# Top-32 attention and two feed-forward layers on one core: rows folded to pairs for the selection, a ScalarE mask, a transposed first layer, and unrolled loops

## The reference

```
scores = scale * np.matmul(q, k.transpose(0, 1, 3, 2))
kth    = np.partition(scores, -32, axis=-1)[..., -32:-31]
scores = np.where(scores >= kth, scores, -1e9)
attn   = np.exp(scores - max); attn = attn / (sum(attn) + 1e-09)
x      = (attn @ v), heads side by side: 2304 x 512
h      = x @ w_in;   y   = (h - tanh(h)) @ w_out            # first layer
h      = y @ w_in2;  out = where(h > 0, h, exp(min(h,0))-1) @ w_out2   # second layer
```

## Time and profile before

| | |
|---|---|
| median of 3 runs | 1284.04 us |
| profiled execution, first to last instruction | 1281.9 us (2.1 us under the median) |
| PE / PEld busy | 94% / 81% |
| DVE / ACT / POOL busy | 70% / 55% / 62% |
| second layer alone, from | 872 us |
| granted TensorE clock, mean | 0.98 |

### The profile page before, as it was taken

One profiled execution on the slowest core, in us unless ns is written; L12 is line 12 of the kernel. 1 busy time (PEld: TensorE's weight loads), 2 busy tenths in 40 slices (PEclk: granted clock), 3 DMA queues, 4 the chain that ended last, 5 costly groups with the idle time before them and its releaser, 6 DMA issues.

```text
span 1281.9 us, 23141 instructions
## 1 busy us (share of the span) xinstructions
PE 1203.8 (94%) x6784; PEld 1039.2 (81%) x6784; DVE 896.5 (70%) x1870; ACT 702.2 (55%) x1534; POOL 790.3 (62%) x579
## 2 busy tenths in 40 slices
PE   3678999999998999999999999999999999999997
PEld 2667887888887888888888888788888888888887
DVE  7999999999999999999999995015532222222221
ACT  5667777766776766777766765345432222222221
POOL 4898888888987888988888986332222222222221
PEclk9679999999999999999999999999999999999999
DMA  6410022000022100022000000504001001010000
GB/s 201 168 56 13 20 62 75 30 21 22 23 68 64 32 21 21 25 66 68 28 26 13 21 11 12 188 12 170 1 1 66 1 1 65 0 50 1 1 33 17
DMA packets 46420, 56.81 MB, mean 44 GB/s; under 512 B 13296, under 2 KB 28656, under 8 KB 45808
## 3 DMA queue, kind: packets, MB, share of 16 engines
q1 hardware_dynamic: 46320, 55.59, 13.7%
HBM read 45.61 MB, written 9.96 MB: 43 GB/s over the span
## 4 chain that ended last, share of the span: by engine, by line
PE 71%; issue 12%; DVE 6%; ACT 5%; POOL 4%; DVEq 0%; DMA 0%; ACTq 0%; POOLq 0%; SPq 0%
PE ps L683 15%; PE ps L728 15%; PE ps L611 11%; PE ps L626 10%; PE ps L598 9%; PE ps L579 4%; PE ps L563 2%; PE ps L564 2%; PE ps L653 2%; DVE best L973 1%; POOL keep L1104 1%; DVE work L1005 1%; DVE best L964 1%; PE ps L580 1%; ACT kT_hi_over_lo L755 1%
## 5 line engine op out<-in xcount | busy, mean ns | idle before, releaser
L1104 POOL TENSOR_SCALAR keep<-scores,best 128x576 f32<-128x576 f32 x144 | 253.6, 1761 | 58.3 <-DVE best L964 55.9
L1148 POOL TENSOR_TENSOR elu_lo<-elu_h,elu_hi 128x512 fp32r<-128x512 f32 x72 | 92.9, 1290 | 305.7 <-ACT elu_hi L755 305.7
L598 PEld LDWEIGHTS ps<-v_and_one,weights_T 128*128 128x128 f32 (+1 forms) x1440 | 183.5, 198 | 56.0 <-issue 49.3
L598 PE MATMUL ps<-v_and_one,weights_T 128*128 128x129 f32 (+2 forms) x1440 | 196.1, 285 | 34.9 <-ACT x L865 33.0
L1110 POOL TENSOR_TENSOR kept_weights<-work,keep 128x576 f32<-128x576 f32 x144 | 205.9, 1430 | 26.8 <-POOL keep L1104 17.8
L964 DVE MAX8 best<-work 128x8 f32<-128x576 f32 x288 | 213.8, 742 | 0.2
L1043 DVE TENSOR_SCALAR exp_h<-exp_h 128x512 f32<-128x512 f32 x72 | 30.7, 427 | 239.9 <-ACT exp_h L907 239.9
L755 ACT ACTIVATE weights_T<-ps 128x512 f32<-128x512 f32 (+1 forms) x288 | 115.1, 433 | 118.6 <-PE ps L580 105.1
L907 ACT ACTIVATE exp_h<-ps 128x512 f32<-128x512 f32 x72 | 43.1, 598 | 194.3 <-PE ps L683 194.3
L821 ACT ACTIVATE work<-scores,exp_bias 128x576 f32<-128x576 f32 x144 | 111.6, 775 | 24.4 <-DVE best L964 24.0
L563 PE MATMUL ps<-kT_hi_over_lo,qT_hi 128*128 128x288 f32 (+1 forms) x320 | 106.1, 347 | 20.1 <-DVE kT_hi_over_lo L937 15.5
(11 more groups left out here) (83 smaller groups left out, 2880.7 us busy)
## 6 DMA issues: line engine op xcount, KB each, us to landing
kT_raw<-kT SPq DMA_DIRECT2D x64, 144.0 KB, 2.8
w_in_raw<-w_in SPq DMA_DIRECT2D x8, 1024.0 KB, 7.5
w_out_raw<-w_out SPq DMA_DIRECT2D x8, 1024.0 KB, 5.5
qT_raw<-qT SPq DMA_DIRECT2D x64, 96.0 KB, 2.5
ffn_rows<-act SPq DMA_DIRECT2D x18, 256.0 KB, 2.1
v_and_one<-v SPq DMA_DIRECT2D x16, 256.0 KB, 2.7
rows<-ffn_rows SPq DMA_DIRECT2D x4, 1024.0 KB, 6.5
out<-out_rows SPq DMA_DIRECT2D x16, 256.0 KB, 2.4
```

The costliest lines, as they stand in the source:

```text
L598: mm = pe.matmul(ps[:, B_OUT, 0:2 * D + 1], pt[0:k, c, :], rhs, start=(c == 0), stop=(c == FULL))
L1104: nc.gpsimd.tensor_scalar(keep[:, :], sc[:, i, :], best[:, i, TOP - 1:TOP], None, ALU.is_ge).then_inc(kept, 1)
```

## The change

Hardware loops are gone. `plan` lists the 144 units (eight heads of a tile, and the four units of a batch's last rows behind its first tile), and every engine's program is one Python loop over slots `s`; slot `s` begins unit `s` on VectorE.

*Selection.* The row is folded: `pair_max` and `pair_min` hold the maximum and the minimum of columns `i` and `i + 288` (two VectorE operations over 288 columns). Of `pair_max` 32 values are drawn (four MAX8, three MATCH_REPLACE8), of `pair_min` 16 (two MAX8, one MATCH_REPLACE8), all on 288 columns. `merge` takes the minimum of the 16 small ones, backwards, and the upper list's last ones, and `rank` takes MAX8 of 17 values, whose eighth is the 32nd largest of the row.

*Mask.* GpSimd makes two biases (minus the 32nd, minus the largest, line 962). ScalarE applies Prelu with slope 1e30 to `score - 32nd` (627), so that what lies below becomes hugely negative, then the exponential in place with its sum (633). VectorE adds the epsilon (844) and inverts (850), GpSimd multiplies the whole row by the inverse (`norm`, 968).

*Products.* The values are the stationary operand (482), two heads in two column halves, which leaves the attended tile already transposed; the copy and the split of it need no transpose. The first layer has hidden columns on the partitions and runs over two tiles (256 tokens): one chunk of 128 hidden columns a slot in slots 24 to 167, 144 chunks; its differences are all on GpSimd (972), its low parts too (977). The second layer's arithmetic is as it was, its weights are loaded and split a block at a time while the last group of the first layer runs.

Core of the diff:

```diff
-                        nc.vector.max(best[:, i, 0:EIGHT], sc[:, i, :]).then_inc(chain_new, 1)
...
-                        nc.gpsimd.tensor_scalar(keep[:, :], sc[:, i, :], best[:, i, TOP - 1:TOP], None, ALU.is_ge
-                                                ).then_inc(kept, 1)
...
-                        nc.gpsimd.tensor_tensor(kept_w[:, :], wk[:, i, :], keep[:, :], ALU.mult).then_inc(masked, 1)
...
+            def upper_max(u, n):
+                if n == 0:
+                    ve.wait_ge(folded, u.t + 1)
+                    after(ve, biased, u.t - 1)
...
+            def fold(u):
+                ve.wait_ge(copied, u.t + 1)
+                nc.vector.tensor_tensor(upper[:, u.t % 2, :], sc[:, u.t % 4, 0:HALF], sc[:, u.t % 4, HALF:S],
+                                        ALU.max).then_inc(folded, 1)
...
+            def biases(u):
+
+                po.wait_ge(ranked, u.t + 1)
+                after(po, exped, u.t - 1)
+                nc.gpsimd.tensor_tensor(bias[:, u.t % 2, :], best[:, u.t % 2, ZERO:ZERO + 2],
+                                        best[:, u.t % 2, TOP8:UPPER + 1:EIGHT], ALU.subtract).then_inc(biased, 1)
+
+            def norm(u):
+                po.wait_ge(inverted, u.t + 1)
+                w = sc[:, u.t % 4, :]
+                nc.gpsimd.tensor_scalar(w, w, rinv[:, u.t % 2:u.t % 2 + 1], 1.0, ALU.mult, ALU.mult).then_inc(normed, 1)
...
+            for s in range(-1, LAST + 1):
+                ranked_u, done = unit(s - 2), unit(s - 5)
+                if ranked_u:
+                    biases(ranked_u)
...
+                if s - 1 in h_in:
+                    difference(h_in[s - 1])
...
+                if ranked_u:
+                    norm(ranked_u)
+                if s - 1 in h_in:
+                    g_low_part(h_in[s - 1])
```

More of the change, by code:

```diff
@@ L34 @@
 LOWEST = -3.0e38
+STEEP = 1.0e30
 EPS = 1e-9
@@ L41, in after, with __init__, plan @@
 def after(eng, sem, count):
-    if not (isinstance(count, int) and count <= 0):
+    if count > 0:
         eng.wait_ge(sem, count)
[L47 to L96, removed]
+class Unit:
+    def __init__(self, t, batch, tile, head=None, pair=None):
+        self.t, self.batch, self.tile, self.head, self.pair = t, batch, tile, head, pair
+        self.tail = head is None
+        self.ends_pair = self.tail or head % 2 == 1
+def plan(batches, per, heads):
+    units = []
+    for b in range(batches):
+        for r in range(per):
+            for h in range(heads):
+                units.append(Unit(len(units), b, b * per + r, head=h, pair=h // 2))
+            if r == 0:
+                for p in range(heads // 2):
+                    units.append(Unit(len(units), b, None, pair=p))
+    return units
 def build(nc, qT, kT, v, w1_in, w1_out, w2_in, w2_out, out):
@@ new lines, in build @@
+    last_unit_of = {u.tile: u.t for u in units if not u.tail}
+    for u in units:
+        if u.tail:
+            last_unit_of[R + u.batch // 2] = u.t
+    tiles = sorted(range(TILES), key=last_unit_of.get)
+    seq_of = {tile: j for j, tile in enumerate(tiles)}
+    RING = 4
+    GN = 2
+    GROUPS = TILES // GN
+    N = GN * P
+    CHUNKS = GROUPS * FC
+    READY = 5
+    h_slot = []
+    for g in range(GROUPS):
+        first = max(last_unit_of[tiles[g * GN + GN - 1]] + READY, h_slot[-1] + 1 if h_slot else 0)
+        h_slot += range(first, first + FC)
@@ new lines, in build @@
+    y_slot = [s + 2 for s in h_slot]
+    LAST = y_slot[-1] + 1
+    LAST_GROUP = (GROUPS - 1) * FC
+    h_in = {s: i for i, s in enumerate(h_slot)}
+    y_in = {s: i for i, s in enumerate(y_slot)}
+    QRING = 3
+    qgroups = []
+    q_of = {}
+    for u in units:
+        if u.tail:
+            q_of[u.t] = (len(qgroups), 0)
+            qgroups.append([u])
+        elif u.head % 2 == 0:
+            q_of[u.t] = (len(qgroups), 0)
+            q_of[u.t + 1] = (len(qgroups), 1)
+            qgroups.append([u, units[u.t + 1]])
@@ L478, in load_tail_tile, with save_y @@
[L478 to L485 removed]
+            def save_y(g, j):
+                tile = tiles[g * GN + j]
+                sp.wait_ge(y_copied, g * GN + j + 1)
+                sp.dma_start(scratch[tile * P:(tile + 1) * P, :], y_rows[:, :]).then_inc(y_saved, DMA)
@@ new lines, in y_step @@
+            def y_step(i):
+                g, f = divmod(i, FC)
+                pe.wait_ge(g_split, i + 1)
+                if f == 0:
+                    after(pe, y_copied, g * GN)
+                if g == 0 and f % CPB == 0:
+                    wait_w1("out", f // CPB)
+                for j in range(GN):
+                    ts = slice(j * P, (j + 1) * P)
+                    for n, (l, r) in enumerate(((gt_hi, wout_hi), (gt_hi, wout_lo), (gt_lo, wout_hi))):
+                        mm = pe.matmul(ps[:, B_Y + j, :], l[:, i % 2, ts], r[:, f, :],
+                                       start=(f == 0 and n == 0), stop=(f == FC - 1 and n == 2))
+                mm.then_inc(y_done, 1)
```

1207 lines of the change are left out of this document (550 added, 657 removed).

## The result

The kernel after takes 1466.84 us (median of 4 runs, 1465.06 to 1467.3) against 1284.2 us (4 runs) of the kernel before on the same chip: a ratio of 1.1423, 95% interval 1.1406 to 1.1441. The forecast was 1487 us, range 1350 to 1570.

The account below looks back on a forecast made before the run. A ring between VectorE and GpSimd, not a busy engine, was taken to bound the attention: 14 start + 145 + 15 + 821 chunk slots + 88 first layer's rest + 402 second layer + 2 = 1487 us, range 1350 to 1570.

Parts of the forecast that it names:

- The ring: VectorE's first MAX8 waits for GpSimd's biases, `norm` for VectorE's reciprocal; 6.84 us a chunk slot, 5.78 without.
- the signs that were to show the ring: VectorE idle 1 us or more before line 806 each slot, VectorE some 75% busy, TensorE near 70%.
- N: Length of GpSimd's `norm`, two multiplications over 576 columns: taken as 1.43 us, range 0.70 to 1.76.
- 5.41 + N: Length of a chunk slot: 5.11 us of steps, 0.3 average port wait, plus `norm`; 6.84 us in all.
- a queries' low part: On GpSimd in every second slot, it holds up VectorE's low fold by 0.63 us, on average 0.3.
- rival 1: Short `norm` of 0.70 us on GpSimd: slots 6.11 us with a chunk, 5.05 without, total 1380 us; chance 0.20.
- The slots ahead of the first chunk: 25 slots at 5.78 us, 145 us, plus 15 us for the weights' low part in front of `norm`.
- The second layer: Unchanged work of 410 us, less 3 for the first layer's last product and 5 for a loop-end stall: 402.
- VectorE's own work: VectorE's folded selection per slot: 5.0 us against 4.9 before, with 0.36 us per 288-column operation.
- Rival 3: VectorE sets the slot, not the exchange with GpSimd: 5.2 us a slot, 1271 us, 1% faster; chance 0.05.
- `norm` blocks nothing: GpSimd's `norm` would not hold up VectorE's folds; by the port rule it would add some 12 us in all.
- Rival 2: Long `norm` of 1.76 us, 1535 us, or TensorE at its lower clock, +40; up to 1575 us; chance 0.26.

Follow-up runs that it names:

- The extra operation: Kernel after plus a useless 512-column GpSimd multiplication in 82 slots: 1517.54 us behind `norm`'s wait, 1476.99 us ahead of it.
- both openings: Kernel after with three list buffers instead of two and GpSimd's low part of a chunk ahead of `norm`: 1406.35 us, 1.0951 of the kernel before.
- the run with the fold put back: The 1274.94 us kernel with the folded selection of the kernel after, in three lists: 1342.67 us, 1.0456 of the kernel before.
- the fastest one: Kernel after with unfolded interleaved selections, three lists, low part first, first-slot edits, and reordering against TensorE's pauses: 1274.94 us, 0.994 of the kernel before.

## Why the prediction was right, and where it wasn't

**The ring: right, in place, form and pieces.** It was to show as VectorE's idle time before line 806, released by `biases`. It does: 69.5 us. From MAX8 to reciprocal 3.57 was predicted, 3.65 measured (mean of the 64 turns in which no low fold is held up, 3.64 to 3.73); biases to MAX8 0.17, measured 0.10; 0.24 to GpSimd, measured 0.10 behind the reciprocal's 0.15; biases 0.22, measured 0.19. The extra operation that counted in full confirms that the ring sets the pace.

**How much of the time is the ring's: less than I laid on it.** The forecast put the whole loss down to the ring and let VectorE alone be about as fast as before. The runs split it otherwise. Of the 183 us over the kernel before, both openings take away 60 (to 1406); the fold, in that frame, is 34 more (to 1373); the order of the selections and the first slots are 59 (to 1314), the pauses with their smaller edit 39 (to 1275). The kernel after would have been slower without its ring too, by 9.5%, so the sign was safer than its reason. Three of the signs that were to show the ring are missing in their size, for the same cause: VectorE's wait is 0.41 us in most slots and not 1 or more, VectorE is busy 88% and not 75, TensorE 84% and not 70. With a short `norm` and a longer selection the ring of 5.8 to 6.2 us lies only 0.5 to 0.7 above VectorE's 5.3 to 5.5.

**N, the length of `norm`: mis-sized.** Taken 1.43, measured 0.745. Both neighbours among the rows misled, the compare with 1.76 and the two-operand multiplication with 1.43; the row far away, a MEMSET scaled to 0.70, was nearly right. Against 5.41 + N = 6.16 the usual slots were 5.79 and 6.22, 6.0 in the mean, so the form of the sum held; a queries' low part costs 0.43 and not 0.63. With the right N the method would have given 1487 - 145 x 0.69 = 1387 us, rival 1; that the total came within 1.4% of the forecast is in part luck. N was too long by 0.69 x 143 = 99 us, and what I had not counted made up for 79 of them:

- Chunk slots that load keys or end a group, 6.5 to 8.5 us, and a low part of 0.93 instead of 0.76: 6.43 in the mean instead of 6.16, 0.27 x 119 = 32 us. The pause of TensorE and its clock behind it belong here.
- The slots ahead of the first chunk: 18 over the forecast, and 17 that the right N would have taken off it, 35 us. Against 24 bare slots of 5.1 us the stretch has 49 us more, of which I had counted 15 for the weights' low part. By experiment 15.5 of the 49 are the queries behind 8 MB of weights, and 9 are the weights' low part in front of `norm` (6 more of it lie in the first chunk slots). The other 25 lie mostly in the first slots (6.2 to 8.3 us), which also prepare the first batch's keys; they weren't tested.
- The second layer, 15 us (the stretch between the last fold and it was 4 less). Of these, 5 are a stall that I had put down to a loop's end: the gap at the end of the chain is still there without loops, 4.32 us at 1450.62. It is the end of the work and not of a loop. Another 9 are the step of 5.57 us instead of 5.44, 72 times, whose cause is open.

**VectorE's own work: wrong by 0.3 to 0.5.** Predicted 5.0 a slot, measured 5.29 and 5.53 with the ring open. A 288-wide MAX8 is 0.36 from start to start as predicted; what was too cheap are the two folds. Beside GpSimd the upper one takes 0.49 to the next start, the lower one up to 0.8 in the usual slots. Rival 3 (faster, VectorE bound, "decides from a slot of 5.3") was thus further off than its 0.05 allowed: with the ring open and everything else mended the folded kernel is 4.6% slower than before, by the run with the fold put back.

**"`norm` blocks nothing": wrong.** I had gone by one pair of rows, `keep` beside a subtraction listed with 0.83. A TENSOR_SCALAR on GpSimd does hold up a two-operand VectorE operation. In the kernel after the upper fold starts while `norm` runs in about 120 of 144 slots; in 100 of these it is listed with 0.56 to 0.57 instead of 0.44 and ends 0.3 us behind `norm`, as the row at 607.92 does:

```profile
607.44 0.75 POOL L968 TENSOR_SCALAR scores<-scores,sum_inverse 128x576 f32<-128x576 f32 x1 [3.31 <-DVE sum_inverse L850]
607.92 0.57 DVE L793 TENSOR_TENSOR pair_max<-scores 128x288 f32<-128x288 f32 x1
```

The low fold was 0.76 instead of 0.44 beside the extra multiplication. And it works the other way too: the chunk's low part is 0.93 where VectorE folds beside it and 0.74 (median) in the runs where it does not. The Trainium skill, "SBUF — State Buffer", section "Who interferes with whom", says that a VectorE instruction with two SBUF inputs contends with a GpSimd instruction that reads SBUF, and one with a single input doesn't. Both are seen here: the folds with two inputs are held up, and the full selection, all of single inputs, ran its MAX8 at 0.74 to 0.76 whatever GpSimd did. On the ring the wait for `norm` cost nothing, as the prediction says of slots with a chunk, since VectorE stood there anyway; with the ring open it is part of the 5.3 to 5.5. The prediction should have let the rule weigh more than one row. Why `keep` held nothing up before (0.82 to 0.83 in eleven of twelve such pairs, against 0.76 with nothing beside it) stays open.

**Rival 2.** Its long `norm` did not come. The lower clock did in part, 0.93 in the mean of the chunk slots, but the usual slots show no cost of it: their wait is the biases'.

**The rest.** TensorE's transposes that went (some 47 us) were not what the kernel after waited for. In the fastest one they would be: TensorE is busy 570 of the 614 us from 150 to 764, and 47 more would not fit. That is an estimate, no run puts them back.

## What to carry to other kernels

Halving the width of a VectorE operation is no saving where it doubles the count and adds operations with two operands; count starts, not listed times, and add what GpSimd does to each two-operand one. Before moving an instruction behind a wait on an in-order engine, follow the token round: a buffer in two copies plus an engine that serves in order is a ring, and its length is the pace even if no engine is busy all the time; a third copy or another order opens it, and what stands behind it (here VectorE's own work) decides how much that gives. Test a ring with one useless operation, once behind the wait and once ahead of it: the difference is the answer.

## Hardware seen that I had not expected

- GpSimd multiplies 576 columns by a value per partition and by a constant in 0.745 us, while a compare with a value per partition over the same columns takes 1.76 and a product of two rows 1.43.
- A 3.00 us pause of TensorE was followed by 3.4 us at half clock in the midst of dense work. Taking away eight pauses of 2.2 to 4.0 us, together with a smaller edit worth some 7 us in the first 24 slots, gave 39 us.
- The same 24 matmuls of 512 columns took 5.44 us a step before and 5.57 after, with starts almost all 0.227 apart before and 0.226 to 0.238 after; moving one operand by 32 or by 64 bytes gave 0.03 to 0.04 back. Open.
